# A fused attention, spectral mixing and MLP kernel: in two batches, pooled rows repeated by DMA and added by VectorE in place of a table product

## The reference

```
q_d, k_d, v_d = means over groups of 4 tokens          # 144 rows a head
out_up    = repeat(softmax(q_d k_d^T / 8) v_d, 4)      # each pooled row stands for 4 tokens
out_local = softmax over |i - j| < 4 of (q k^T / 8) v
x = out_up + out_local                                 # heads side by side: 576 x 512
```

## Time and profile before

| | us |
|---|---|
| median of 3 runs | 764.14 |
| lowest and highest | 763.96, 766.54 |
| the profiled execution's own time | 765.54 |
| its span, first to last instruction | 763.7 |

### The profile page before, as it was taken

The page is one execution under the profiler, slowest core; times in us unless marked ns, Lnnn a source line. Parts: engine busy times, 40 slices in busy tenths (PEclk is TensorE's granted clock), DMA queues, the critical chain, the costliest instruction groups (busy, mean ns, idle before and its releaser), DMA issues.

```text
span 763.7 us, 14781 instructions
## 1 busy us (share of the span) xinstructions
PE 715.4 (94%) x5960; PEld 540.7 (71%) x5960; DVE 382.2 (50%) x925; ACT 193.6 (25%) x417; POOL 151.6 (20%) x131
## 2 busy tenths in 40 slices
PE   2579959999999998999999999999999999999998
PEld 1455646877767876877767877877767877777776
DVE  4457585554555852543555873543555851123452
ACT  1536531322212122222212132222212121111201
POOL 8001677991101211000201311000101300000000
PEclk9999858999999999999999999999999999999999
DMA  9994228022001036022000127022000000000001
GB/s 264 283 254 123 85 88 199 19 66 64 11 1 58 21 102 160 2 59 64 18 2 32 39 78 193 2 59 66 16 1 1 9 29 27 1 2 1 1 23 40
DMA packets 42246, 48.96 MB, mean 64 GB/s; under 512 B 4803, under 2 KB 35846, under 8 KB 41094
## 3 DMA queue, kind: packets, MB, share of 16 engines
q1 hardware_dynamic: 32608, 31.06, 16.0%
q10 hardware_dynamic: 9574, 16.99, 7.3%
HBM read 43.32 MB, written 4.72 MB: 63 GB/s over the span
## 4 chain that ended last, share of the span: by engine, by line
PE 85%; DVE 4%; DMA 3%; POOL 3%; issue 2%; ACT 2%; ACTq 1%; SPq 0%; POOLq 0%
PE Y L580 24%; PE P L563 24%; PE Y L685 4%; PE P L696 4%; PE P L685 4%; PE A L592 3%; PE Y L696 3%; PE A L646 2%; PE A L550 2%; DMA out<-ot 2%; PE A L543 2%; PE A L533 2%; PE A L635 1%; PE A L486 1%; PE P L543 1%
## 5 line engine op out<-in xcount | busy, mean ns | idle before, releaser
L563 PE MATMUL P<-unT,w_wv 128*128 128x288 f16 x1536 | 212.0, 289 | 3.9 <-DVE hT L1144 3.1
L580 PE MATMUL Y<-hT,w 128*128 128x288 f16 x1536 | 215.2, 287 | 0.0
L563 PEld LDWEIGHTS P<-unT,w_wv 128*128 128x128 f16 x1536 | 149.6, 99 | 49.1 <-issue 6.4
L1144 DVE SCALAR_TENSOR_TENSOR hT<-P,hT 128x288 f16<-128x288 f32 x128 | 58.4, 457 | 248.9 <-ACT hT L820 248.5
L580 PEld LDWEIGHTS Y<-hT,w 128*128 128x128 f16 x1536 | 146.3, 98 | 42.1 <-issue 5.3
L820 ACT ACTIVATE hT<-P 128x288 f16<-128x288 f32 x128 | 52.4, 411 | 212.3 <-PE P L563 210.7
L1180 DVE SCALAR_TENSOR_TENSOR gate<-xT,cw,gate 128x288 f32<-128x288 f32 x128 | 66.4, 519 | 4.5
L791 ACT ACTIVATE prob_or_un<-prob_or_un 73x288 f32<-73x288 f32 (+1 forms) x52 | 23.3, 448 | 88.5 <-DVE prob_or_un L1017 84.8
L1315 POOL MEMSET x<- 1x512 f32 x4 | 2.1, 517 | 209.0 <-ACT x L809 209.0
L696 PE MATMUL Y<-shared,wo 128*128 128x288 f32 x128 | 32.1, 409 | 0.5 <-DVE shared L1190 0.5
L696 PE MATMUL P<-shared,wo 128*128 128x288 f32 x128 | 31.8, 407 | 0.5 <-DVE shared L1190 0.5
(11 more groups left out here) (167 smaller groups left out, 839.3 us busy)
## 6 DMA issues: line engine op xcount, KB each, us to landing
kl<-qk_win SPq DMA_DIRECT2D x38, 140.0 KB, 6.5
ql<-qk_win SPq DMA_DIRECT2D x19, 256.0 KB, 4.4
vl<-v_win SPq DMA_DIRECT2D x72, 65.0 KB
pair_or_folded<-qk_pool SPq DMA_DIRECT2D x8, 580.0 KB, 5.8
pair_or_spectrum<-qk_pool SPq DMA_DIRECT2D x8, 580.0 KB, 6.3
out<-ot ACTq DMA_DIRECT2D x32, 144.0 KB, 1.8
w_wv<-w_ch ACTq DMA_DIRECT2D x4, 1024.0 KB, 11.7
w<-w_ch ACTq DMA_DIRECT2D x4, 1024.0 KB, 11.0
```

The costliest lines, as they stand in the source:

```text
L563: last = mm(P[s % 2][:, 0:HN], w1s(k, f, wt), unT[:, ut, k, ha * HN:(ha + 1) * HN], start=k == 0 and wt + ut == 0, stop=k == KD - 1 and wt ...
L580: last = mm(Y[d][:, 0:HN], w2s(f, d, wt), hT[s % 3][:, ht, :], start=f == 0 and wt + ht == 0, stop=f == KF - 1 and wt == 1)
L1144: nc.vector.scalar_tensor_tensor(out=hT[s % 3][:, 1, :], in0=P[s % 2][:, 0:HN], scalar=0.0, in1=hT[s % 3][:, 0, :], op0=ALU.max, op1=ALU.s ...
```

## The change

In the batches b = 2 and 3 the table product is left out, and the first of the sixteen values products on each part of the bank starts it anew. GpSimd issues DMAs that read the pooled rows of `xd` four times each and write them into `x` (`repeat_pooled`): for units 0 and 1 as soon as all pooled rows are there, for units 2 and 3 after the wait for unit 2's keys and queries, for unit 4 after the wait for unit 3's. They are twelve DMAs a batch: one each for units 0 and 1, two, three and five for units 2, 3 and 4. VectorE then adds the bank to `x` (`unit_add`), in place of ScalarE's copy, and waits for these DMAs through a semaphore for each unit, `ld_up`. Batches 0 and 1 keep the table.

```diff
@@ -194,6 +194,7 @@
         normed = sem("normed")
         spread_made = sem("spread_made")
         x_sb = sem("x_sb")
+        ld_up = [sem(f"ld_up{t}") for t in range(NT)]
         x_zeroed = sem("x_zeroed")
         fold_a = sem("fold_a")
@@ -297,6 +298,21 @@
             if opening(b):
                 return ql[i][:], kl[i][:], ld_qk[i], (1, 1, 1, 2, 2)[t]
             return ql[i][:], kl[i][:], ld_qk[i], b * (3 - i) + t // 2 + i
+        def by_table(b):
+            return isinstance(b, int) and b <= 1
+        def pooled_rows(t):
+            if t < 2:
+                return [(0, 128, t, 0, 32 * t, 32)]
+            if t == 2:
+                return [(1, 125, 3, 1, 0, 31), (125, 128, 3, 1, 31, 1)]
+            if t == 3:
+                return [(0, 1, 4, 1, 31, 1), (1, 125, 4, 1, 32, 31), (125, 128, 4, 1, 63, 1)]
+            return [(0, 32, 2, 0, 64, 8), (32, 33, 2, 0, 72, 1), (0, 1, 5, 1, 63, 1), (1, 29, 5, 1, 64, 7), (29, 32, 5, 1, 71, 1)]
         def unit_at(b, m, s, lag):
@@ -534,21 +550,22 @@
                                       vd[:, k, u, :], start=k == 0, stop=k == 1)
                 else:
                     t = u - UD
-                    if t == 0:
-                        pe.wait_ge(normed, UD * (b + 1))
-                        if not later(b):
-                            pe.wait_ge(spread_made, 2)
-                    for tile, lo, r in ([(LOCAL_TILE[t], 0, 128)] if t < 4 else [(2, 0, 2 * LQ), (5, 2 * LQ, 2 * LQ)]):
-                        first = 128 * (tile % 3) + (1 if tile < 3 else 0)
-                        mm(R[lo:lo + r, :], spread[:, first:first + r], xd[:, tile // 3, :], start=True, stop=False, skip_group_check=True)
-                    if opening(b):
-                        pe.wait_ge(probT_done, n + 1)
+                    if by_table(b):
+                        if t == 0:
+                            pe.wait_ge(normed, UD * (b + 1))
+                            if opening(b):
+                                pe.wait_ge(spread_made, 2)
+                        for tile, lo, r in ([(LOCAL_TILE[t], 0, 128)] if t < 4 else [(2, 0, 2 * LQ), (5, 2 * LQ, 2 * LQ)]):
+                            first = 128 * (tile % 3) + (1 if tile < 3 else 0)
+                            mm(R[lo:lo + r, :], spread[:, first:first + r], xd[:, tile // 3, :], start=True, stop=False, skip_group_check=True)
+                        if opening(b):
+                            pe.wait_ge(probT_done, n + 1)
                     V, landed, count = values(b, t)
                     pe.wait_ge(landed, 128 * count)
                     for i in range(4):
                         for w in range(4):
                             last = mm(R[LQ * w:LQ * w + LQ, :].rearrange("p (j i d) -> p j i d", j=2, i=4)[:, :, i], PT[0:2 * LK, i * 128 + LQ * w:i * 128 + LQ * w + LQ],
-                                      V[:, w // 2 + 2 * (w % 2), :, i, 0:D], start=False, stop=True, skip_group_check=True)
+                                      V[:, w // 2 + 2 * (w % 2), :, i, 0:D], start=not by_table(b), stop=True, skip_group_check=True)
                 last.then_inc(av_done, 1)
             def mlp_up(b, s):
@@ -938,7 +955,7 @@
                         for u in unit_at(b, m, s, LAG_T):
                             unit_probT(b, u)
                     for u in unit_at(b, m, s, LAG_AV):
-                        if u >= UD:
+                        if u >= UD and by_table(b):
                             unit_out(b, u)
                     if m is None:
                         for c in W1_HIGH.get(s, []):
@@ -1045,6 +1062,17 @@
                 tt(xd[:, :, u * D:(u + 1) * D], R[0:GQ, 0:2 * (D + 1)].rearrange("p (g c) -> p g c", g=2)[:, :, 0:D],
                    rz[0:GQ, 1, 0:2].unsqueeze(2).to_broadcast([GQ, 2, D]), ALU.mult).then_inc(normed, 1)
+            def unit_add(b, u):
+                t = u - UD
+                dve.wait_ge(av_done, b * NU + u + 1)
+                dve.wait_ge(ld_up[t], 16 * len(pooled_rows(t)) * (b - 1))
+                R = banks(b, u)[2]
+                for tile, lo in [(LOCAL_TILE[t], 0)] if t < 4 else [(2, 0), (5, 2 * LQ)]:
+                    r = XROWS[tile]
+                    last = tt(x[0:r, tile, :], R[lo:lo + r, :], x[0:r, tile, :], ALU.add)
+                last.then_inc(x_sb, 1)
             def fold(b, i):
                 r = ROWS[i]
@@ -1216,6 +1244,8 @@
                             if u > UD or m is not None:
                                 unit_shift(b, u)
                         if m is not None:
+                            for u in unit_at(b, m, s, LAG_AV) if not by_table(b) else []:
+                                unit_add(b, u)
                             for u in pair_at(b, s, 0):
                                 unit_shift(b, u)
                                 unit_shift(b, u + 1)
@@ -1318,6 +1348,19 @@
                     if t in FOLD_AFTER:
                         fold_even(b, FOLD_AFTER.index(t))
+            def repeat_pooled(b, t):
+                if t == 0:
+                    pool.wait_ge(normed, UD * (b + 1))
+                    pool.sem_inc(passed, 1)
+                if t in (2, 4):
+                    _, _, landed, count = keys(b, t // 2 + 1)
+                    pool.wait_ge(landed, 48 * count)
+                    pool.sem_inc(passed, 1)
+                for lo, hi, tile, rev, first, groups in pooled_rows(t):
+                    src = xd[first:first + groups, rev, :].unsqueeze(1).to_broadcast([groups, (hi - lo) // groups, DM])
+                    pool.dma_start(x[lo:hi, tile, :], src).then_inc(ld_up[t], 16)
             def fold_even(b, i):
                 r = ROWS[i]
                 pool.wait_ge(x_sb, NT * b + FOLD_AFTER[i] + 1)
@@ -1348,6 +1391,9 @@
                     for c in range(2, WCH):
                         second_weights(c)
                     pool.wait_ge(w2_split, WCH)
+                if not by_table(b):
+                    for i in range(NT):
+                        repeat_pooled(b, i)
                 zero_rows(b)
                 if opening(b):
                     pool.wait_ge(w_scale, 2)
```

## The result

| | before | after |
|---|---|---|
| median of 6 runs each, us | 765.70 | 758.21 |
| lowest and highest | 763.96, 769.85 | 757.01, 760.35 |
| the profiled execution's own time | 765.54 | 760.19 |
| its span | 763.7 | 758.3 |

The ratio of after to before is 0.9884, 95% interval 0.9855 to 0.9914. On 765.70 us that is a gain of 8.9 us, between 6.6 and 11.1; the two medians by themselves differ by 7.5. The forecast was 755.2 on a median of 764.14, a ratio of 0.988. The kernel is about 1% faster, clear of the noise, and its time lies in the forecast's range.

The account below looks back on a forecast made before the run. TensorE was taken as the bound, 85% of the chain of waits. Profiled 765.54 less 9.0 for tables plus 0.1 for slot 17 gave 756.6, or 755.2 on the median 764.14; 8-in-10 range 753.7 to 759.0.

Parts of the forecast that it names:

- TensorE's part: Table products dropped from TensorE in two batches: 4.45 to 4.90 us saved a batch, 4.5 taken, 9.0 in all.
- VectorE's part: Bank additions replacing ScalarE's copies: 0.66 us each in VectorE's queue, 4 us a batch, almost no cost to the kernel.
- Slot 17, the tight one: VectorE's xT additions there start 0.5 us late, with 0.26 us still to spare: cost 0, bound 0.3 a batch.
- GpSimd's part: Twelve DMA issues a batch on GpSimd's queue, 1.2 us each taken, all out ahead of its memsets.
- The start behind unit 2's keys: GpSimd's issues for units 2 and 3 wait for these keys, forecast to land at some 338 us.
- The margin to the memset: GpSimd's last copy issues, unit 4's five, are out by 350, 12 us ahead of its memsets.
- The room of the DMA engines: A batch's 1.2 MB of copies takes 3.3 us at 361 GB/s, so the engines have room.
- Rival 1: Units 2 and 3: a 124-row copy on one engine, 11.0 us, comes late; 759 to 764 us, chance 9%.
- it fits by 7 us: One-engine copies of units 2 and 3 land at 351 and 362, needed by 358.8 and 369.4, if alone on the engine.
- Rival 2: Start of the fourth batch's slots: a longer wait and low clock, +1.5 + 1.7 us, 758.4; chance 10%.
- Rival 3: Issuing on GpSimd's queue is the bound, delaying sums and VectorE's fold; at 3.5 us an issue 772; chance 5%.
- the likeliest case: Whole kernel, the forecast without rivals: 755.2 us, own range 754.0 to 756.5, chance 76%.

Follow-up runs that it names:

- `no_up`: The changed kernel without copies or additions; pooled rows left out in b = 2 and 3, ScalarE copies the bank; 757.38 us, ratio 0.9892 to before.
- `add_only`: The changed kernel without copies or the wait for them; VectorE adds the bank to old rows of x; 758.6 us, ratio 0.9903 to before.
- Experiment 4: The changed kernel with VectorE's additions but no copies, old rows of x standing in for the pooled ones; 758.6 us, ratio 0.9903 to before.
- experiment 2: The changed kernel with neither copies nor additions, the pooled rows missing from x in b = 2 and 3; 757.38 us, ratio 0.9892 to before.
- `three_early`: The changed kernel with b = 1 also without tables, two copies ahead of the last weights and ten behind; 764.74 us, ratio 0.9983 to before.
- `three_singles`: The changed kernel with three-row copies made as one-row copies and b = 1 also without tables; 764.45 us, ratio 0.9971 to before.
- The second set of runs: The changed kernel, unaltered, timed again beside the kernel before; 759.1 us against 765.85, ratio 0.991.
- experiment 8: The changed kernel with ScalarE issuing the twelve copies in its slots 10, 12, 14 and 16; 773.1 us, ratio 1.0082 to before.

## Why the prediction was right

**TensorE's part, 4.45 to 4.9 a batch, taken 4.5.** Right, and right at its lower end: 4.46 (after), 4.45 (`no_up`), 4.44 (`add_only`), always for b = 3. This is the mechanism that the forecast rests on. The 0.09 us of the tile switch is not saved; it moved from the table to the values product. Taking all of 0.95 a unit would have been 0.4 a batch too much.

**VectorE's part.** Right. The addition is 0.69 us long and 0.60 in the queue, against 0.66 used. Slot 17, the tight one, cost nothing: the xT additions stand 0.5 us late as worked out, and the spare time held. Experiment 4 has the same net step as experiment 2, which has no addition.

**GpSimd's part.** Right in order and outcome, too high in price: 0.72 us an issue where 1.2 was taken. The start behind unit 2's keys was forecast at 338 on the scale of before; it is 341.41, less the 3.56 us by which this step starts later (292.06 against 288.50), 337.85. The margin to the memset is 9.9 us; 12 was forecast.

**The room of the DMA engines.** Wrong. It did little harm because the copies are issued early enough. The prediction reckoned 1.2 MB as 3.3 us of all engines' 361 GB/s. Half a megabyte of it runs on one engine a copy and takes until 358.3. It looked for a wait of VectorE for the copies, and of GpSimd's successors, but not at what the copies do to the loads beside them. SyncE's issues of the values stretch from 6.8 to 10 or 11 us, their data land 3.5 to 4.9 us later still, and the values product waits 0 to 1.1 us a batch. The forecast has 0.1 us a kernel for slot 17; the values wait there is 0.65 in one execution and 2.16 in the other, by another cause.

**Rival 1** (a copy carried by one engine, 9%) did come, and only its price did not. Its 11.0 us a copy are somewhat low: each chain of packets takes 12 to 13 us beside the other loads, the first from 343.88, the second from 346.35, and both are through at 358.3. Its "two engines if the copies are on different ones" is what happened, so they end at 357.4 and 358.9 in place of 351 and 362. Unit 2's addition started at 361.81, 4.4 us later, and unit 3's at 370.16, 11 us later. The prediction had "it fits by 7 us". So its sign, a wait of the additions for x<-xd, was absent although its condition held, and the 759 to 764 us did not follow; in `three_early` and `three_singles`, where GpSimd starts late, they do wait. The Trainium skill ("DMA: Bandwidth & Descriptors", section "Why a DMA increments its semaphore by 16 and not by 1") has a rule under which 31 groups against 124 rows share only the divisor 1 and stay on one engine, with an exception for some GpSimd copies. These traces agree with the rule, and the exception does not apply to these copies. The semaphore steps (30 of 32 by 348.25, the last two behind 357) and the two chains of packets are the evidence.

**Rival 2** came in small: +0.48 us at the start of the fourth batch's slots and no low clock; over the executions of this study that wait was 0.70 to 2.40, and before has 0.78. **Rival 3** did not come.

**The absolute time.** 758.21 lies 3.0 us above the 755.2 forecast and outside the likeliest case's own range of 754.0 to 756.5. Half of it is that before's median is 765.70 with six runs in place of three. The rest is that the medians differ by 7.5 us and 8.9 was forecast. The ratio's interval (6.6 to 11.1) holds both, and so it cannot tell them apart. The second set of runs, 6.75 between the medians, lies on the side of 7.5, and the waits for late values, 1.4 us a kernel in the mean of the two traces, are of that size. So the mechanism of the gain was right, and a loss of about a microsecond and a half was not in the sum.

**What stays open.** How the large copies make SyncE's issues and the values' data late. All kernels with the copies have the longer issues, and none without them has. The engines were not full (a busy share of 0.47 in 344 to 355, which a mean of 16 engines can show with two of them loaded all the time), and the issue that follows a one-engine copy on ScalarE is held for 3.9 to 5.9 us. Both fit the thought that a load which needs the two loaded engines has to stand behind them. But no run here shows on which engines the parts of a load run, and no variant spreads the 124 rows over more engines. That is the obvious next trial. No variant that computes the whole result beat the changed kernel.

## What to carry to other kernels

Work taken from a saturated TensorE is worth the distance of its starts less what its neighbour takes over, here the 0.09 us switch of tile shape; read it where a neighbour of the same shape stands. A DMA that is small against the bandwidth can still delay others: look at how many engines carry it, how long the issues beside it take and which load is next late, not at bytes. Where several copies share a semaphore, a time from issue to landing that a view gives for each of them may belong to another; look at the last step of the semaphore. And judge such a change by cutting the span into steps, since an untouched first stretch that varies by over 5 us hides or feigns half of a 9 us gain, and look at the granted clock in each step before taking its length for the change's.

## What was not expected of the hardware

**A copy of 128 rows spreads over the engines and one of 124 rows does not.** 256 KB are complete 3.9 and 5.7 us after the issue, 248 KB 15 to 16 us after it. The first move on up to 18 packets at once, the second in one chain each. They differ in the number of rows (32 groups of four against 31) and in the loads that run beside them.

**The issue behind such a copy holds ScalarE's queue**, for 3.9 to 5.9 us, where GpSimd needs 0.72 an issue (experiment 8).

**GpSimd's sum stops a tiny VectorE operation.** L1044, 8 elements a partition, takes 0.17 us in 14 of 20 places of after. In slot 19 it takes 0.97 and ends at 372.23; GpSimd's sum of two SBUF tiles ends at 372.20:

```profile
370.93 1.27 POOL L1369 TENSOR_TENSOR fa<-x 128x512 f32<-128x512 f32 x1 [5.85 <-DVE x L1073]
```

It is 1.04 us in `add_only` too, where GpSimd issues no DMA (sum from 368.75 to 370.02, L1044 from 369.00 to 370.04):

```profile
369.00 1.04 DVE L1044 TENSOR_SCALAR lz<-mx 128x8 f32<-128x8 f32 x1
```

In before the same operation was done at 370.19, ahead of the sum at 371.37, and took 0.17. With the addition on VectorE the sum is released 0.1 us after it and meets the scaling. The Trainium skill, "SBUF — State Buffer", section "SBUF: two separate sides", says that VectorE in a two-port mode and GpSimd take a shared pair of ports in turn, each for a whole instruction. The two ends that fall together agree with it. Here the 0.8 us lay in spare time and cost nothing.
